# Attention, a token-mixing perceptron and a gated output in float32: three blocks of engine programs joined into one, with the last steps of the attention reordered around the first mixing

## The chip, the cores and the metric

The kernel runs on one core of a Trainium2 chip. The metric is the time of one execution on the device in microseconds (us); lower is better. The engines are named as in the profile: PE (matmuls and transposes), DVE, ACT and POOL for the elementwise work, SP as issuer of most DMAs.

## What is computed

The reference, cut to what matters. Shapes: q, k, v (4, 8, 576, 64), x (4, 576, 512), U (576, 32), V (32, 576), w_ch1 (512, 2048), w_ch2 (2048, 512), w_val and w_out (512, 512), conv_w (5, 512).

```python
scores = q @ k.T / sqrt(64)
scores = where(scores >= max(scores) - tau, scores, -1e9)
attn = exp(scores - max(scores)); attn = attn / (sum(attn) + 1e-9)
x = (attn @ v)                                   # back to (4, 576, 512)

u = x + (x.T @ U @ V).T                          # mixing of the tokens
x = u + maximum(u @ w_ch1, 0) @ w_ch2            # perceptron

gate = sigmoid(sum(conv_w[j] * xp[:, j:j + 576] for j in range(5)))
out = (gate * (x @ w_val)) @ w_out
```

## The kernel before

Everything is float32. A product is made of three matmuls of parts: an operand is split into a high part (rounded to the matmul's format) and a low part (the rest), and high x high, high x low and low x high are added in PSUM. The high parts are casts on ACT, the low parts subtractions on DVE or POOL. The tokens stay transposed on the chip in `x_t`, 128 channels on the partitions in four column blocks d for each of 4 batches. Each batch has two halves of 288 tokens (`CHUNK`).

The kernel is three functions, each with one block of five engine programs. A block ends for all engines together. Every engine runs its own instructions in the order written; between engines there are semaphores (`until` and `wait_ge` wait, `then_inc` counts).

`attention` goes through 80 steps m (`STEPS`: 16 pairs of heads, 5 blocks of query rows: 128, 128, 128, 96, 96) and 160 scores n = 2m, 2m + 1. For a step PE makes the scores (`score_rows`), transposes the weights (`transpose_main(m, a)`, `transpose_tails(m)`) and multiplies them with v (`weigh_values(m)`, L291); ACT makes exponentials (L369) and evacuates the transposes (`evac_main`, L396, `evac_tails`, L402); DVE makes the maximum (L494), the thresholded weights (`weights`, L503) and `normalise(m)` into `x_t` (L516). POOL splits q and k and, one chunk for each pair, makes the low part of w1 (`w1_low`, L227). PSUM has eight banks: scores take banks 0 to 5 in turn, the transposes bank 6, the output of `weigh_values` bank 7.

Behind the last scores comes the drain, L343 to L360 on PE, where the first mixing (batch 0, first half) is woven in: `transpose_tokens(k)` (L304) brings five blocks of tokens of batch 0 into banks 2 to 5 as scores leave them, ACT and DVE split them (`token_high` L412, `token_low` L522), `mix_down(k)` multiplies them with U (`u4_sb`, L315 and L316) into bank 0, `g_high` (L459) and `g_low` (L541) split the result g, `mix_up(d)` (L326) multiplies it with V, `mix_sum(d)` (L548) adds it to x. `u_high` is L463, the low parts of u are made by POOL (L237, d = 0, 1) and DVE (L580, d = 2, 3). `u4_sb` and V (`v4_sb`) are split in the drain too.

`mixing_and_perceptron` has 32 units u for each of the 4 batches, 16 for each half. A unit on PE is `hidden(b, u)` (L721 to L723, 12 matmuls with w1) and `output(b, u - 1)` (L736 to L738, 12 matmuls with w2, `h_used` counts them); `hidden_high` on ACT (L787) and `hidden_low` on DVE (L862) stand between them. Row blocks 0 to 8 of w2 are in `w2a_hi` and `w2a_lo`, the other seven in `w2b_hi` and `w2b_lo`; they are loaded and split one by one in the first 16 units (`w2_high` L799, `w2_low` L875). In the last batch w_val and w_out are split into freed places, and `x_high` (L808) and `x_low` (L888) make the parts of the first two chunks of x. POOL makes the convolution of each chunk (18 steps, L932 and L936) and SP stores it to DRAM (`conv_dram`).

`gated_output` has eight chunks c of 288 tokens. PE runs `value(c)` (48 matmuls, L1005 to L1007) into banks 0 to 3 and then two or three `project(s)` (12 matmuls of 512 columns, L1020 to L1022). SP loads `gates`, ACT makes `sigmoid(c)` (L1055), DVE `multiply(c)` (L1083, four), ACT `gated_high(c)` (L1043), DVE `gated_low(c)` (L1088). `x_high(c + 2)` (L1037) and `x_low(c + 2)` (L1076) prepare the chunk after the next. POOL makes the convolution of the last chunk beside this. On DVE the order of a chunk is:

```python
            for c in range(CHUNKS):
                multiply(c)
                if c + 2 < CHUNKS:
                    x_low(c + 2)
                gated_low(c)
```

## Time and profile before

| | |
|---|---|
| runs shown (3) | 835.25, 836.61, 836.88 us; median 836.61 |
| profiled execution | 835.42 us; span of its instructions 833.6 us |
| granted PE clock, mean over the span | 0.998 |
| busy, share of the span | PE 98%, DVE 53%, ACT 48%, POOL 48% |
| HBM | 38.81 MB read, 8.85 MB written, 57 GB/s over the span |

The span goes from the first to the last instruction of the profiled execution; the execution's own time is 1.8 us longer. The attention takes the first 36% of the span, the perceptron goes to 87%. The page says who is busy, the waits say who waited for whom, the timelines show each instruction with the idle time before it, and the windows show busy time and clock of a stretch. A matmul's recorded duration (0.29 us for 288 columns) is longer than its distance to the next (0.133 us), since matmuls overlap; costs on PE are counted from start to start. "PEq" is PE's sequencer, which is what the waits name where a block begins.

### The profile page before, as it was taken

What the parts mean: (1) busy time and instruction counts of PE and PEld (TensorE: products, weight loads), DVE (VectorE), ACT (ScalarE), POOL (GpSimd) and SP (SyncE); (2) the same over time, 40 slices, a digit from 0 to 9 for tenths busy, and PEclk for the clock granted to TensorE, in tenths of its full rate; (3) what the DMA queues carried; (4) which work ended last, traced back from release to release, by engine and by line L of the source; (5) the groups of instructions that cost most, each with busy time, mean ns of one, the idle gap of its engine ahead of it and who ended that gap; (6) DMA issues with size and microseconds to landing.
All of it is one profiled execution on the core that took longest, in us unless ns stands there. A gap on an engine that the chain in (4) does not pass through costs nothing. (4 is left out here: it accounts for less than half of the span.)

```text
span 833.6 us, 17430 instructions
## 1 busy us (share of the span) xinstructions
PE 812.9 (98%) x6864; PEld 770.5 (92%) x6864; DVE 443.4 (53%) x996; ACT 397.4 (48%) x1019; POOL 396.6 (48%) x290
## 2 busy tenths in 40 slices
PE   4999999999999989999999999999999999999998
PEld 4889888899889879999999999999999999988986
DVE  6999999999999854332231322313223123384231
ACT  5999999999999933222121221212212112244231
POOL 4999887788860000082280731905509147191000
PEclk9999999999999999999999999999999999999999
DMA  7444334333422022100000000000000102122221
GB/s 180 115 128 115 85 110 125 104 85 93 125 64 69 2 64 89 39 1 29 1 29 2 1 29 1 2 29 1 29 2 1 54 25 82 37 104 94 80 79 63
DMA packets 27759, 49.36 MB, mean 59 GB/s; under 512 B 5344, under 2 KB 14112, under 8 KB 27680
## 3 DMA queue, kind: packets, MB, share of 16 engines
q1 hardware_dynamic: 24944, 43.54, 18.5%
q10 hardware_dynamic: 2736, 4.72, 1.5%
q8 instruction: 55, 0.90, 0.4%
q14 instruction: 24, 0.20, 0.1%
HBM read 38.81 MB, written 8.85 MB: 57 GB/s over the span
## 5 line engine op out<-in xcount | busy, mean ns | idle before, releaser
L862 DVE SCALAR_TENSOR_TENSOR h_lo<-psum,h_hi 128x288 fp32r<-128x288 f32 x128 | 58.6, 458 | 244.7 <-ACT h_hi L787 244.7
L787 ACT ACTIVATE h_hi<-psum 128x288 fp32r<-128x288 f32 x128 | 52.7, 412 | 256.0 <-PE psum L723 256.0
L721 PE MATMUL psum<-u_split,w_hi 128*128 128x288 f32 x512 | 152.0, 297 | 3.1 <-PEq L135 3.1
L723 PE MATMUL psum<-u_split,w_lo 128*128 128x288 f32 x512 | 152.3, 297 | 0.0
L722 PE MATMUL psum<-u_split,w_hi 128*128 128x288 f32 x512 | 151.8, 297 | 0.0
L494 DVE TENSOR_REDUCE neg_max<-psum 128x1 f32<-128x576 f32 (+1 forms) x160 | 119.2, 745 | 20.4 <-PE psum L254 20.1
L503 DVE SCALAR_TENSOR_TENSOR probs<-psum,thresh,exp_scores 128x576 f32<-128x576 f32 (+1 forms) x160 | 129.3, 808 | 0.8 <-ACT exp_scores L369 0.8
L932 POOL TENSOR_TENSOR conv<-x_t,cw 128x576 f32<-128x576 f32 x14 | 16.1, 1153 | 232.5 <-DVE x_t L870 231.9
L369 ACT ACTIVATE exp_scores<-psum,neg_max 128x576 f32<-128x576 f32 (+1 forms) x160 | 118.1, 738 | 0.0
L253 PE MATMUL psum<-qk_split 128*128 128x288 f32 (+1 forms) x320 | 105.8, 345 | 10.5 <-DVE qk_split L482 9.6
L721 PEld LDWEIGHTS psum<-u_split,w_hi 128*128 128x128 f32 x512 | 97.1, 190 | 3.9 <-issue 3.3
L722 PEld LDWEIGHTS psum<-u_split,w_hi 128*128 128x128 f32 x512 | 96.9, 189 | 0.7
L723 PEld LDWEIGHTS psum<-u_split,w_lo 128*128 128x128 f32 x512 | 96.9, 189 | 0.0
L254 PE MATMUL psum<-k_lo,qk_split 128*128 128x288 f32 (+1 forms) x320 | 91.5, 300 | 0.0
L396 ACT COPY probs_t<-psum 128x384 f32<-128x384 f32 (+2 forms) x160 | 79.5, 497 | 13.9 <-PE psum L264 12.3
L737 PE MATMUL psum<-h_lo,w2a_hi 128*128 128x288 f32 x288 | 85.1, 296 | 0.0
L736 PE MATMUL psum<-h_hi,w2a_hi 128*128 128x288 f32 x288 | 85.1, 295 | 0.0
L738 PE MATMUL psum<-h_hi,w2a_lo 128*128 128x288 f32 x288 | 85.0, 295 | 0.0
L264 PE MATMUL psum<-ident,probs 128*128 128x128 f32 (+1 forms) x560 | 82.6, 264 | 0.8 <-ACT probs_t L396 0.8
L936 POOL TENSOR_TENSOR conv<-conv,term 128x576 f32<-128x576 f32 x56 | 81.0, 1447 | 4.4
L291 PE MATMUL psum<-probs_t,v_main 128*64 128x128 f32 (+1 forms) x1280 | 80.7, 268 | 0.0
L253 PEld LDWEIGHTS psum<-qk_split 128*128 128x128 f32 (+1 forms) x320 | 58.3, 182 | 23.1 <-issue 16.5
(127 smaller groups left out, 1900.4 us busy)
## 6 DMA issues: line engine op xcount, KB each, us to landing
qk_raw<-in_qk SPq DMA_DIRECT2D x60, 288.0 KB, 4.3
out<-o_sb ACTq DMA_DIRECT2D x18, 256.0 KB, 2.0
w_stage<-in_w SPq DMA_DIRECT2D x16, 256.0 KB, 3.1
v_main<-in_v SPq DMA_DIRECT2D x16, 256.0 KB, 2.6
conv<-in_w SPq DMA_DIRECT2D x16, 256.0 KB, 2.6
conv_dram<-conv SPq DMA_DIRECT2D x7, 576.0 KB, 2.9
gates<-conv_dram SPq DMA_DIRECT2D x7, 576.0 KB, 3.7
probs<-in_qk SPq DMA_DIRECT2D x4, 288.0 KB, 5.0
```

The lines of the kernel that those rows point to most:

```text
L253: nc.tensor.matmul(out, split[:, hd, 0, rows], split[:, hd, 1, cols], start=True, stop=False)
L254: mm = nc.tensor.matmul(out, split[:, hd, 0, rows], k_lo[:, hd, cols], start=False, stop=True)
L264: mm = nc.tensor.transpose(psum[:, T_BANK, kb * P:kb * P + rows], probs[0:rows, m % 3, at:at + P], ident[0:rows, 0:rows])
L369: nc.scalar.activation(halves(e_sb[0:rows, n % 2]), scores(n, rows), ACT.Exp, bias=neg_max[0:rows, n % 5:n % 5 + 1]).then_inc(exp_done, 1)
L494: nc.vector.tensor_reduce(neg_max[0:rows, n % 5:n % 5 + 1], scores(n, rows), AX.XY, ALU.max, negate=True).then_inc(max_done, 1)
L503: nc.vector.scalar_tensor_tensor(out=halves(probs[0:rows, m % 3, n % 2 * S:(n % 2 + 1) * S]), in0=scores(n, rows), scalar=thresh[0:rows, n ...
L721: nc.tensor.matmul(out, w1_hi[:, cols], u_hi[:, half, d], start=(d == 0), stop=False)
L722: nc.tensor.matmul(out, w1_hi[:, cols], u_lo[:, half, d], start=False, stop=False)
L723: mm = nc.tensor.matmul(out, w1_lo[:, cols], u_hi[:, half, d], start=False, stop=(d == DB - 1))
L736: nc.tensor.matmul(out, hi[:, cols], h_hi[:, u % 2], start=(f == 0), stop=False)
L737: nc.tensor.matmul(out, hi[:, cols], h_lo[:, u % 2], start=False, stop=False)
L738: mm = nc.tensor.matmul(out, lo[:, cols], h_hi[:, u % 2], start=False, stop=(f == FB - 1))
```

## The change

- The three functions return their engine programs, and one block runs them one behind the other, so each engine goes on to the next function when it is itself done. Waits that the blocks' ends gave are written out as semaphores.
- In the drain, the token transposes stand ahead of the last steps' transposes; the order on PE, ACT and DVE is new. The last two scores' work on ACT is taken out of the loop. `mix_down` runs in two column halves of 256 into banks 0 and 1, `g_high` and `g_low` likewise, and `mix_up(0)` waits for the first half alone. `hidden(0)` waits for each column block of the low part of u. All low parts of u are made on DVE. `weigh_values(78)` comes behind `mix_up`; `transpose_tails(79)`, `weigh_values(79)`, `evac_tails(79)` and `normalise(79)` go into the first two units of the perceptron.
- U and V are split on POOL, ahead of its last `w1_low`, with products by one in place of ACT's casts. `g4_sb` and `tok_lo` swap their places, the ring of `probs` is shifted by one. The loads of w2 wait for the split of V.
- `gates` lies in the place of the first rows of `w2b_hi`; its first two loads wait until these rows have been used for the last time (`h_used`) and run within the perceptron.
- `value(0)` writes banks 4 to 7, `value(1)` waits for `x2_done`. `gated_high(c)` stands ahead of `x_high(c + 2)` and `gated_low(c)` ahead of `x_low(c + 2)`. POOL's last convolution waits for `x_low(2)`.

The diff, cut to its core; the shift of the bodies' indentation is left out.

```diff
+Programs = namedtuple("Programs", "sync gpsimd tensor scalar vector")
+LastStep = namedtuple("LastStep", "transpose_tails weigh_values evac_tails normalise")
...
     tok_hi, tok_lo = parts[0:5], parts[5:10]
-    X_BANKS, G_BANK = [2, 3, 4, 5, 2], 0
+    X_BANKS, G_BANKS, G_COLS = [2, 3, 4, 5, 2], [0, 1], [slice(0, DM // 2), slice(DM // 2, DM)]
+    U_BANKS = [0, 2, 3, 1]
...
             work(p)
-        for c in (PAIRS - 2, PAIRS - 1):
-            pool.wait_ge(w1_lo_done, c)
-            w1_low(c)
-        for d in (0, 1):
-            pool.wait_ge(u_hi_done, d + 1)
-            nc.gpsimd.tensor_tensor(*low_part_of_u(d), ALU.subtract)
+        pool.wait_ge(w1_lo_done, PAIRS - 2)
+        w1_low(PAIRS - 2)
...
+        pool.wait_ge(mix_in, 16 * 5)
+        pool.wait_ge(w1_lo_done, PAIRS - 1)
+        u_rank, v_rows = slice(0, 3 * RANK), slice(RANK, 2 * RANK)
+        nc.gpsimd.tensor_tensor(u4_sb[:, :, u_rank], u4_raw[:, :, u_rank],
+                                one[:].unsqueeze(2).broadcast_to([P, 5, 3 * RANK]), ALU.mult).then_inc(u4_hi_done, 1)
+        pool.wait_ge(u4_hi_done, 1)
+        nc.gpsimd.tensor_tensor(u4_sb[:, :, 3 * RANK:P], u4_raw[:, :, 3 * RANK:P], u4_sb[:, :, 0:RANK].bitcast(F32),
+                                ALU.subtract).then_inc(u4_ready, 1)
+        pool.wait_ge(u4_ready, 1)
+        nc.gpsimd.tensor_tensor(v4_sb[:], v_stage, one[:].broadcast_to([P, S]), ALU.mult).then_inc(v_hi_done, 1)
+        pool.wait_ge(v_hi_done, 1)
+        nc.gpsimd.tensor_tensor(v4_sb[v_rows], v_stage[v_rows], v4_sb[v_rows].bitcast(F32), ALU.subtract
+                                ).then_inc(v_split, 1)
+        pool.wait_ge(v_split, 1)
+        w1_low(PAIRS - 1)
...
             pe.wait_ge(tok_evac, k + 1)
-            nc.tensor.matmul(psum[:, G_BANK, :], u4_sb[0:rows, k], tok_hi[k][0:rows], start=(k == 0), stop=False)
-            mm = nc.tensor.matmul(psum[:, G_BANK, :], u4_sb[0:rows, k], tok_lo[k][0:rows], start=False,
-                                  stop=(k == 4))
-            if k == 4:
-                mm.then_inc(g_sum, 1)
+            for bank, cols in zip(G_BANKS, G_COLS):
+                out = psum[:, bank, 0:DM // 2]
+                nc.tensor.matmul(out, u4_sb[0:rows, k], tok_hi[k][0:rows, cols], start=(k == 0), stop=False)
+                mm = nc.tensor.matmul(out, u4_sb[0:rows, k], tok_lo[k][0:rows, cols], start=False, stop=(k == 4))
+                if k == 4:
+                    mm.then_inc(g_sum, 1)
...
             if d == 0:
-                pe.wait_ge(g_ready, 1)
                 pe.wait_ge(v_split, 1)
-            nc.tensor.matmul(psum[:, 2 + d, 0:CHUNK], g4_sb[:, d * P:(d + 1) * P], v4_sb[:, 0:CHUNK],
+            pe.wait_ge(g_ready, d // 2 + 1)
+            nc.tensor.matmul(psum[:, U_BANKS[d], 0:CHUNK], g4_sb[:, d * P:(d + 1) * P], v4_sb[:, 0:CHUNK],
                              start=True, stop=True).then_inc(mix_ready, 1)
...
             score_rows(2 * i + 1)
+            if i == STEPS - 1:
+                transpose_tokens(0)
+                transpose_tokens(1)
             if i > 1:
                 transpose_main(i - 2, 1)
-                transpose_tails(i - 2)
+                transpose_tails(pe, i - 2)
             if i + 1 < STEPS:
                 score_rows(2 * i + 2)
+            else:
+                transpose_tokens(2)
+                transpose_tokens(3)
             if i > 0:
...
             if i > 1:
-                weigh_values(i - 2)
+                weigh_values(pe, i - 2)
-        transpose_tokens(0)
-        transpose_tokens(1)
-        transpose_main(STEPS - 2, 1)
-        transpose_tails(STEPS - 2)
-        transpose_tokens(2)
-        transpose_main(STEPS - 1, 0)
-        weigh_values(STEPS - 2)
-        transpose_tokens(3)
-        mix_down(0)
         transpose_tokens(4)
-        mix_down(1)
-        transpose_main(STEPS - 1, 1)
-        transpose_tails(STEPS - 1)
-        for k in (2, 3, 4):
+        mix_down(0)
+        transpose_main(STEPS - 2, 1)
+        transpose_tails(pe, STEPS - 2)
+        for k in range(1, 5):
             mix_down(k)
-        weigh_values(STEPS - 1)
+        transpose_main(STEPS - 1, 0)
         for d in range(DB):
             mix_up(d)
+        weigh_values(pe, STEPS - 2)
+        transpose_main(STEPS - 1, 1)
...
-        for i in range(STEPS):
+        def g_high(c):
+            act.wait_ge(g_sum, c + 1)
+            nc.scalar.copy(g4_sb[:, G_COLS[c]], psum[:, G_BANKS[c], 0:DM // 2]).then_inc(g_hi_done, 1)
+        def u_high(d):
+            act.wait_ge(u_sum, d + 1)
+            nc.scalar.copy(high_part_of_u(d), u_cols(d)).then_inc(u_hi_done, 1)
+        for i in range(STEPS - 1):
...
-        spread_inverse(STEPS - 2)
-        act.wait_ge(mix_in, 16 * 5)
-        nc.scalar.copy(u4_sb[:, :, 0:3 * RANK], u4_raw[:, :, 0:3 * RANK]).then_inc(u4_hi_done, 1)
+        spread_inverse(STEPS - 3)
+        threshold(2 * STEPS - 2)
+        exponent(2 * STEPS - 2)
+        guard_sums(STEPS - 2)
+        w1_high(PAIRS - 1)
         token_high(0)
+        threshold(2 * STEPS - 1)
+        exponent(2 * STEPS - 1)
         token_high(1)
-        evac_main(STEPS - 2, 1)
-        evac_tails(STEPS - 2)
+        evac_main(STEPS - 3, 1)
+        evac_tails(act, STEPS - 3)
         guard_sums(STEPS - 1)
         token_high(2)
-        evac_main(STEPS - 1, 0)
-        spread_inverse(STEPS - 1)
+        evac_main(STEPS - 2, 0)
+        spread_inverse(STEPS - 2)
         token_high(3)
         token_high(4)
-        nc.scalar.copy(v4_sb[:], v_stage).then_inc(v_hi_done, 1)
-        evac_main(STEPS - 1, 1)
-        evac_tails(STEPS - 1)
-        act.wait_ge(g_sum, 1)
-        nc.scalar.copy(g4_sb[:], psum[:, G_BANK]).then_inc(g_hi_done, 1)
+        evac_main(STEPS - 2, 1)
+        evac_tails(act, STEPS - 2)
+        spread_inverse(STEPS - 1)
+        evac_main(STEPS - 1, 0)
+        act.wait_ge(w1_lo_done, PAIRS)
+        g_high(0)
+        g_high(1)
         for d in range(DB):
+            u_high(d)
+        evac_main(STEPS - 1, 1)
...
+        def u_low(d):
+            dve.wait_ge(u_hi_done, d + 1)
+            nc.vector.tensor_tensor(u_split[:, 0, 1, d], u_cols(d), high_part_of_u(d).bitcast(F32),
+                                    ALU.subtract).then_inc(u_low_done, 1)
...
-        weights(2 * STEPS - 1)
-        normalise(STEPS - 3)
-        u4_low()
         token_low(0)
+        weights(2 * STEPS - 1)
         token_low(1)
...
         token_low(2)
-        normalise(STEPS - 2)
+        normalise(dve, STEPS - 3)
         token_low(3)
         token_low(4)
-        v_low()
-        g_low()
-        normalise(STEPS - 1)
-        for d in range(DB):
-            mix_sum(d)
-        for d in (2, 3):
-            dve.wait_ge(u_hi_done, d + 1)
-            nc.vector.tensor_tensor(*low_part_of_u(d), ALU.subtract)
+        g_low(0)
+        g_low(1)
+        mix_sum(0)
+        mix_sum(1)
+        u_low(0)
+        mix_sum(2)
+        u_low(1)
+        mix_sum(3)
+        normalise(dve, STEPS - 2)
+        u_low(2)
+        u_low(3)
...
+    (gates,), (w2b_hi,) = overlay(nc, ctx, [("gates", [P, 2, DB, CHUNK], F32)], [("w2b_hi", [P, FB - FA, DM], F32R)])
...
+    def sync(sp):
+        sp.wait_ge(v_split, 1)
         for f in range(1, FB):
...
                 until(pe, g_ready, b)
+            if b == 0 and d == 0:
+                pe.wait_ge(o_evac, STEPS)
...
             until(pe, h_done, n - 1)
+            if b == 0 and half == 0 and f % DB == 0:
+                pe.wait_ge(w1_lo_done, PAIRS - DB + f // DB + 1)
             out = psum[:, 4 + u % 2, 0:CHUNK]
             for d in range(DB):
+                if n == 0:
+                    pe.wait_ge(u_low_done, d + 1)
...
                 hidden(b, u)
+                if first and u == 0:
+                    last_step.transpose_tails(pe, STEPS - 1)
+                if first and u == 1:
+                    last_step.weigh_values(pe, STEPS - 1)
...
             until(act, w2_in[f % 2], 16 * ((f + 1) // 2))
+            if f == FA:
+                act.wait_ge(o_evac, STEPS)
             nc.scalar.copy(w2_rows(w2a_hi, w2b_hi, f), w2_stage[f % 2]).then_inc(w2_hi_done, 1)
...
                 hidden_high(b, u)
+                if first and u == 0:
+                    last_step.evac_tails(act, STEPS - 1)
...
+        act.wait_ge(mix_in, 16 * 5)
         w2_high(0)
...
                 hidden_low(b, u)
+                if first and u == 1:
+                    last_step.normalise(dve, STEPS - 1)
...
     BLOCKS = B * S // P
+    x2_done, h_used, conv_out, first_x_ready = perceptron_sems
+    VALUE_BANK = [4] + [0] * (CHUNKS - 1)
...
+    def sync(sp):
         for c in range(CHUNKS):
...
             until(sp, gv_part, DB * (c - 1))
+            if c < 2:
+                last_row = ((c + 1) * DB * CHUNK - 1) // DM + FA
+                sp.wait_ge(h_used, (CHUNKS - 1) * (FB - 1) + last_row + 1)
             if c == CHUNKS - 1:
...
             else:
+                sp.wait_ge(conv_out, 16 * (c + 1))
                 sp.dma_start(gates[:, c % 2], conv_dram[c]).then_inc(gate_in[c % 2], 16)
...
+    def gpsimd(pool):
+        pool.wait_ge(x_ready, DB)
+        pool.wait_ge(x2_done, CHUNKS * DB)
         convolution(nc, pool, B - 1, 1, 0, x_t, last_conv, term, cw, conv_step)
...
             for d, k in itertools.product(range(DB), repeat=2):
-                until(pe, x_ready, (c - 2) * DB + k + 1)
-                if k == 0:
-                    until(pe, gv_part, (c - 1) * DB + d + 1)
-                out_ps, cols = psum[:, d, 0:CHUNK], slice(k * DM + d * P, k * DM + d * P + P)
+                if c > 1:
+                    pe.wait_ge(x_ready, (c - 2) * DB + k + 1)
+                else:
+                    pe.wait_ge(first_x_ready, 2 * k + c + 1)
+                if k == 0 and c > 1:
+                    pe.wait_ge(gv_part, (c - 1) * DB + d + 1)
+                if k == 0 and c == 1:
+                    pe.wait_ge(x2_done, (CHUNKS - 1) * DB + d + 1)
+                out_ps, cols = psum[:, VALUE_BANK[c] + d, 0:CHUNK], slice(k * DM + d * P, k * DM + d * P + P)
...
         for c in range(CHUNKS):
+            gated_high(c)
             if c + 2 < CHUNKS:
                 x_high(c + 2)
-            gated_high(c)
...
             multiply(c)
+            gated_low(c)
             if c + 2 < CHUNKS:
                 x_low(c + 2)
-            gated_low(c)
...
+            gated = gated_output(nc, stage, w_val_hi, w_val_lo, (w2a_hi, w2a_lo), cw, conv_dram, out, psum, x_t, gates,
+                                 perceptron_sems)
+            with nc.Block() as block:
+                @block.sync
+                def _(sp):
+                    scores_and_values.sync(sp)
+                    perceptron.sync(sp)
+                    gated.sync(sp)
```

## Rows read from the trace of the kernel before

**Rows 1.** Page, part 1: busy us (share of the span) xinstructions of each engine.

```profile
PE 812.9 (98%) x6864; PEld 770.5 (92%) x6864; DVE 443.4 (53%) x996; ACT 397.4 (48%) x1019; POOL 396.6 (48%) x290
```

**Rows 2.** Waits of PE: line waited for, us in total, times, longest us.

```profile
PE psum L253 <- DVE qk_split L482: 9.6, 2, 8.4
PE psum L721 <- PEq L135: 3.1, 1, 3.1
PE psum L1020 <- DVE gv_lo L1088: 2.0, 1, 2.0
```

**Rows 3.** Timeline, PE, 725 to 742: start us, us, instruction, [idle before <-releaser].

```profile
725.14 0.29 PE L738 MATMUL psum<-h_hi,w2b_lo 128*128 128x288 f32 x1
726.25 0.37 PE L1005 MATMUL psum<-w2a_hi,w_val_hi 128*128 128x288 f32 x1 [0.82 <-PEq L640]
...
738.98 0.29 PE L1007 MATMUL psum<-w2a_hi,w_val_lo 128*128 128x288 f32 x1
741.24 0.50 PE L1020 MATMUL psum<-w2a_hi,gv_hi 128*128 128x512 f32 x1 [1.97 <-DVE gv_lo L1088]
```

**Rows 4.** Timeline, PE, 282 to 304, the drain and the first unit.

```profile
282.62 0.49 PE L264 MATMUL psum<-ident,probs 128*128 128x128 f32 x3
...
289.62 0.48 PE L315 MATMUL psum<-qk_split,u_sb 128*128 128x512 f32 x1
...
290.17 0.60 PE L304 MATMUL psum<-ident,x_t 128*64 128x128 f32 x4
...
293.28 0.88 PE L291 MATMUL psum<-probs_t,v_main 128*64 128x96 f32 x16
...
294.75 0.80 PE L326 MATMUL psum<-v_sb,g_sb 128*128 128x288 f32 x4 [0.42 <-DVE g_sb L541]
298.60 0.37 PE L721 MATMUL psum<-u_split,w_hi 128*128 128x288 f32 x1 [3.06 <-PEq L135]
...
303.39 0.29 PE L736 MATMUL psum<-h_hi,w2a_hi 128*128 128x288 f32 x1
```

**Rows 5.** Windows: us, busy us (x) of PE, PEld, DVE, ACT, POOL, clock, DMA, GB/s.

```profile
284.00:286.00 2.00, 2.00 (x28) 1.71 (x28) 1.35 (x6) 2.00 (x7) 0.77 (x1) 1.00 0.00 0
300.00:301.00 1.00, 1.00 (x6) 1.00 (x5) 0.00 (x0) 0.00 (x0) 0.00 (x0) 0.50 0.82 207
330.00:400.00 70.00, 70.00 (x526) 69.55 (x525) 22.66 (x45) 16.42 (x36) 22.91 (x18) 1.00 0.08 25
```

**Rows 6.** Timeline, DVE, 294 to 298.

```profile
294.00 0.69 DVE L541 TENSOR_TENSOR g_sb<-psum,g_sb 32x512 fp32r<-32x512 f32 x1 [1.12 <-ACT g_sb L459]
...
296.87 1.42 DVE L580 TENSOR_TENSOR u_split<-x_t,u_split 128x288 fp32r<-128x288 f32 x2
```

**Rows 7.** Timeline, POOL, 283 to 298.

```profile
283.49 1.28 POOL L227 TENSOR_TENSOR w_lo<-w_stage,w_hi 128x512 fp32r<-128x512 f32 x1 [15.80 <-ACT w_hi L407]
296.19 1.79 POOL L237 TENSOR_TENSOR u_split<-x_t,u_split 128x288 fp32r<-128x288 f32 x2 [11.42 <-ACT u_split L463]
```

**Rows 8.** Timeline, DVE, 733 to 757.

```profile
733.38 5.59 DVE L1076 TENSOR_TENSOR w2a_lo<-x_t,w2a_hi 128x288 fp32r<-128x288 f32 x4
738.89 2.30 DVE L1088 TENSOR_TENSOR gv_lo<-gv,gv_hi 128x1152 fp32r<-128x1152 f32 x1
...
754.02 1.56 DVE L1076 TENSOR_TENSOR w2a_lo<-x_t,w2a_hi 128x288 fp32r<-128x288 f32 x4
756.08 1.36 DVE L1088 TENSOR_TENSOR gv_lo<-gv,gv_hi 128x1152 fp32r<-128x1152 f32 x1 [0.50 <-ACT gv_hi L1043]
```

**Rows 9.** Timeline, ACT, 293 to 298.

```profile
293.38 0.59 ACT L459 CAST g_sb<-psum 128x512 fp32r<-128x512 f32 x1 [0.84 <-PE psum L316]
295.68 1.52 ACT L463 CAST u_split<-x_t 128x288 fp32r<-128x288 f32 x4 [1.71 <-DVE x_t L548]
```

**Rows 10.** Timeline, ACT, 726 to 731.

```profile
726.50 1.28 ACT L1055 ACT_TABLE_LOAD   x1 [3.14 <-PEq L640]
730.16 1.17 ACT L1055 ACTIVATE gates<-gates 128x1152 f32<-128x1152 f32 x1 [2.38 <-DMA gates<-conv_dram]
```

More of the change, by code:

```diff
@@ new lines, in gpsimd, with convolve, batch @@
+    def gpsimd(pool):
+        def convolve(b, half):
+            c = b * 2 + half
+            if isinstance(b, int) and c == 0:
+                pool.wait_ge(w2_ready, FB)
+            pool.wait_ge(x2_done, c * DB + DB)
+            until(pool, conv_out, c * 16)
+            convolution(nc, pool, b, half, c * CONV_STEPS, x_t, conv, term, cw, conv_step)
+        def batch(b, first, last):
+            if not first:
+                convolve(b - 1, 1)
+                pool.wait_ge(conv_step, b * (2 * CONV_STEPS))
+            convolve(b, 0)
+        batch_loop(batch)
```

1307 lines of the change are left out of this document (643 added, 664 removed).

## The prediction

> **What bounds the kernel now.** I read the page first. PE is busy for 812.9 us of a span of 833.6 [rows 1], so only its idle time and its slow stretches can be won; DVE, ACT and POOL are busy for about half. The waits of PE name the idle time: 3.1 us before the first matmul of the perceptron (L721), 2.0 before the first output projection (L1020) [rows 2], 0.82 before the first value matmul (L1005) [rows 3], 0.42 before the first `mix_up` (L326) [rows 4]. Most of the rest of the span's 20.7 us without PE is the start (8.4 us until the first scores [rows 2]) and the last store, both left alone by the change. The windows show one thing more: just behind the 3.1 us gap the granted clock is 0.50 (1.2 of 2.4 GHz), while it is 1.00 before and later [rows 5]. Then I took the timelines around the two places where one block ends and the next begins, near 295 us and near 725 us; everything the change can move lies there. In between, one unit of the perceptron is 24 matmuls at 0.133 us from start to start (526 in 70 us of an always busy PE [rows 5]), and the change adds nothing to it.
>
> **First place: attention to perceptron.** `output(0)`, the first matmul of w2, starts at 303.39 [rows 4]. I compute when it starts after the change.
>
> Old order. `score_rows(159)` is the last instruction on PE that both orders share; what follows it starts at 282.62 [rows 4]. From there to `mix_up(0)` at 294.75 PE has 12.1 us, of which I add up 10.6 us of work (start to start: 0.33 to 0.46 for a group of transposes, 1.25 or 0.98 for `weigh_values` with 128 or 96 rows, 0.55 for one `mix_down`, 289.62 to 290.17 in [rows 4]) and 1.5 of waits. From `mix_up(0)` to the first matmul of `hidden(0)` are 3.85 us (294.75 to 298.60): DVE and ACT have to make u, its high and its low part for four column blocks, POOL makes two of the low parts while DVE makes the others, and both are slow at it (1.42 us for two on DVE, 1.79 on POOL [rows 6, 7]), where DVE takes 1.56 for four of this shape when POOL rests [rows 8]; then the blocks' barrier, 0.3 us, since DVE ends at 298.29. From 298.60 to `output(0)` are 4.79 us for 24 matmuls. At 0.133 they would take 3.2, or 3.3 with a slow first one; the other 1.5 us are what the low clock costs.
>
> New order. Before `mix_up(0)` PE no longer has `weigh_values(78)` (0.98), `transpose_main(79,1)` (0.25), `transpose_tails(79)` (0.25) and `weigh_values(79)` (0.98): 10.6 - 2.5 = 8.1 us. The ten matmuls of `mix_down` with 512 columns become twenty with 256. Bounds: 0.11 us each (a transpose of 128 columns) to 0.24 (one of 512 columns); I take 0.14, near the 0.133 of 288 columns plus what a change of weights adds in `mix_down` now, so 2.8 us as before (2.2 to 4.7). Waits in the new order: `transpose_tokens(2)` for the weights of score 158 (0.3), `transpose_main(78,0)` for ACT, which now has two `token_high` and one exponential ahead of its evacuation (0.3), a slow first matmul behind each wait (0.3 in all), and the chain ahead of `mix_up(0)`: `evac_main(79,0)` stands in front of `g_high(0)` on ACT (0.37 us from start to start), then the halves of `g_high` and `g_low`. These took 0.59 and 0.69 with 512 columns [rows 6, 9], four casts of 288 took 1.52, so about 0.43 for one; I take 0.43 for each half (0.3 to 0.69), with hops 1.6 us. So `mix_up(0)` starts at 282.6 + 8.1 + 0.9 + 1.6 = 293.2.
>
> From there DVE has the chain: `mix_sum(0)` starts 0.45 later, and eight instructions of 0.37 us from start to start, `normalise(78)` of 0.26 in their midst and a wait of 0.2 for `u_high(0)` end with `u_low(3)` at 297.1; POOL is idle, so none is slowed. PE takes `weigh_values(78)` and `transpose_main(79,1)` (1.2 us) meanwhile and runs the first three quarters of `hidden(0)` as the low parts come, since its waits are now one for each column block. The last three matmuls start at 297.1 and leave PE free at 297.5. `transpose_tails(79)`, `hidden(1)` and `weigh_values(79)` follow (0.25 + 1.6 + 0.98 = 2.8), so `output(0)` starts at 300.3: 3.1 us earlier than 303.39. This counts the clock as kept: no single wait in this stretch is longer than 1.6 us, and the old kernel has one of 1.97 us at 739 with full-speed matmuls behind it [rows 3], while its fall came behind one of 3.06.
>
> Edits at no cost, and their cover. The splits of u4 and v4 leave ACT and DVE for POOL. POOL is idle for 15.80 us ahead of its last `w1_low` [rows 7], and four instructions of 0.5 to 1.4 us each, some 4 us, fit in there; their five loads stand in SP's queue as before, ahead of the last load of w1, and POOL waits for them with nothing but the last `w1_low` queued behind. The last `w1_low` must now be done before ACT's `g_high`: it ends near 285. SP's loads of w2 wait for the split of v4 and so start well before the perceptron. `normalise(79)` stands behind `hidden_low(1)` on DVE and holds back `w2_low(2)` by under 1 us; `output(2)` needs that more than 5 us later. The shifted ring of `probs` moves no instruction.
>
> **Second place: perceptron to gated output.** The last matmul of the perceptron starts at 725.14, the first of `value(0)` at 726.25: 1.11 us, where 0.13 is the pitch. The last of `value(1)` starts at 738.98, `project(0)` at 741.24: 2.26 us, where 0.13 is the pitch [rows 3]. With 0.1 for each slow first matmul, both gaps are 3.2 us. What ends the second is DVE: `x_low(2)` stands ahead of `gated_low(0)`, and POOL's last convolution runs beside them; four `x_low` take 5.59 us and `gated_low` 2.30, where later chunks show 1.56 for the four and 1.36 for `gated_low` [rows 8]. New: `value(0)` writes banks 4 to 7, free once `hidden_low(31)` has read, which the last `output` waits for anyway, so it follows at 725.3 and `value(1)` ends at 738.1. The gates load while PE is in units 12 to 14 (from about 713, some 4 us each), so ACT takes its table (1.28 us) and the first sigmoid (1.17) right behind its last `x_high`; ACT has been idle for 3.14 us at 726.50, so that is from 723.4, and both are done near 726, ahead of the first value block at 727. Now the sigmoid starts at 730.16 [rows 10]. `multiply(0)` ends at 732.3, `gated_high(0)` at 733.5 and, with POOL still waiting for `x_ready`, `gated_low(0)` at 734.9. `project(0)` wants it at 738.1: cover of 3.2 us, both gaps go, 3.2 us.
>
> What comes due later. POOL's 18 steps start near 737 instead of 726 and end near 765, so the slow DVE instructions move into chunks 1 and 2. For a chunk these are 2.6 + 5.7 + 4 x 0.46 = 10.1 us of DVE in 12.0 us of PE; `x_low(3)` ends near 748 and `value(3)` wants it at 756, `x_low(4)` at 760 for 768. Covered by some 8 us; `last_conv` is read only by the last chunk.
>
> **Sum.** 3.1 + 3.2 = 6.3 us. The profiled execution took 835.42 (span 833.6); less 6.3 that is 829.1. The median of the runs is 836.61, 1.2 above the profiled one; by it the time is 830.3. I take 829.8.
>
> **Rivals.**
> - *The clock falls in the drain all the same.* For it: the new order puts six groups of transposes together from 282.6 to 286, and PE then idles in five pieces until 297. Against: the whole attention stage with its transposes is at 1.00, and so is the old drain up to the 3.06 us gap. Price: as now 1.5 us, 831.3. The Trainium skill, "TensorE: Matmul & The Clock Gate", Part 4, says that transposes don't count as busy work for the clock gate as matmuls do; by it this rival would be the forecast and the drain would be slow at that place. Of the trace of before a mixed window bears on it, against the rule: 284 to 286, with value matmuls and token transposes, is at 1.00 [rows 5]; a pure run of transposes of 3 us it does not have. Chance 0.12.
> - *The chain on ACT and DVE eats the gain of the drain.* A half of g or an evacuation costs more than I took, or PE's extra matmuls cost 0.24 each (+1.9 us), and `output(0)` starts only 1 us or less earlier. Only the second place pays: 832. Chance 0.12.
> - *The second place keeps its gap*, because the gates or the semaphores of the last w2 rows come late, or DVE waits for PE at `x2_done`: 2 us back, 831.8. The first sigmoid has 2 to 6 us of cover. Chance 0.06.
> - *Slower.* POOL's later convolution meets DVE where DVE is on PE's path. DVE has 10.1 us of work in 12.0; if each slowed instruction takes twice the 1.4 and 2.6 us, DVE falls 6 to 8 us behind in each of two chunks, its 8 us of cover are gone in the second, and PE loses more than the 6.3 gained: about 838. It decides from some 16 us of DVE a chunk. The price of the slowed instructions is measured beside the same POOL instructions, so it is unlikely. Chance 0.03.
>
> **Chances and range.** The forecast holds 0.67. About 0.2% is what a measurement of this kernel can tell from no change: 1.7 us, and every case but the last is well below 835: faster 0.93, same 0.04 (the first two rivals together with the third), slower 0.03. Low end: the profiled time less both gains, with 1.3 us more from cheaper halves and an earlier u, 827.8. High end: the first and second rivals and some scatter of the runs, 832.6.
>
> **What would show it.** In the profile after: no `PEq` wait before the first w1 matmul; clock 1.00 in each window from 282 to 305; the first `mix_down` halves at 0.14 us; about 1.5 us of PE's wait before the first `mix_up`; `output(0)` near 300.3; no wait of PE between 720 and 745 beyond 0.2 us; the four `x_low` of chunk 2 at 1.6 us and those of chunk 3 at 5.7, with PE unbroken. A slow stretch of matmuls between 286 and 300, or an idle PE at `value(3)`, would make the prediction wrong.

## The result, and the profile after

The changed kernel takes 829.37 us (median of 4 runs, 829.22 to 830.13) against 836.75 us for the kernel before, a ratio of 0.9921 (95% interval 0.9909 to 0.9933). Five more runs on another occasion gave 829.30 (829.24 to 829.33) and a ratio of 0.9924 [0.9911, 0.9936]. The forecast was 829.8, its range 827.8 to 832.6. The span of the profiled execution fell from 833.6 to 827.3, so by 6.3 us, where 6.3 was predicted; 0.2 us of that were there when the scores ended, as shown below.

The page's span and busy line, and then the waits of PE (engine, tensor, line waited at, what ended it, us in total, times, longest), of the changed kernel:

```profile
span 827.3 us, 17448 instructions
...
PE 811.4 (98%) x6874; PEld 769.3 (93%) x6874; DVE 440.8 (53%) x997; ACT 396.1 (48%) x1018; POOL 398.9 (48%) x292
...
engine line waited for: us in total, times, longest us
PE psum L309 <- DVE qk_split L515: 9.6, 2, 8.4
PE psum L355 <- DVE g_sb L556: 1.4, 1, 1.4
PE psum L309 <- DVE probs L536: 0.9, 1, 0.9
PE psum L320 <- DVE probs L536: 0.3, 1, 0.3
PE psum L320 <- ACT probs_t L423: 0.2, 1, 0.2
PE psum L749 <- DVE u_split L561: 0.2, 1, 0.2
```

PE is busy 1.5 us less although it has ten matmuls more, which fits the 1.5 us that the low clock cost before. The waits of 3.1 and 2.0 us [rows 2] are gone; of waits over 1 us only one is left behind the start, 1.4 us ahead of the first `mix_up` (L355).

The first place, PE's timeline from the end of the scores to `output(0)` (start, us, engine, line, operation, tensors, shapes, count, the idle time before and what ended it):

```profile
282.27 0.30 PE L310 MATMUL psum<-k_lo,qk_split 128*96 128x288 f32 x1
282.40 1.04 PE L332 MATMUL psum<-ident,x_t 128*128 128x128 f32 x8
...
287.81 0.28 PE L346 MATMUL psum<-qk_split,u_sb 128*128 128x256 f32 x1
287.92 0.28 PE L345 MATMUL psum<-qk_split,u_sb 128*128 128x256 f32 x1
...
290.87 0.55 PE L320 MATMUL psum<-ident,probs 96*128 96x96 f32 x4
292.81 0.78 PE L355 MATMUL psum<-v_sb,g_sb 128*128 128x288 f32 x4 [1.39 <-DVE g_sb L556]
293.52 0.88 PE L166 MATMUL psum<-probs_t,v_main 128*64 128x96 f32 x16
...
294.78 0.37 PE L749 MATMUL psum<-u_split,w_hi 128*128 128x288 f32 x1
...
296.31 0.41 PE L749 MATMUL psum<-u_split,w_hi 128*128 128x288 f32 x1 [0.23 <-DVE u_split L561]
```

`output(0)` starts at 300.19 (row below), where it was at 303.39 [rows 4]: 3.2 us earlier. The scores ended 0.22 us earlier already (282.40 against 282.62), which is scatter: in the profiles of the two kernels and their variants they end between 282.24 and 282.99. Counted from there, `output(0)` comes after 17.79 us in place of 20.77, so the drain itself gives 2.98. The halves of `mix_down` follow each other at 0.11 to 0.13 us, and at 0.20 behind a change of weights. `hidden(0)` now begins at 294.78, 3.8 us before its old 298.60, and takes its column blocks one by one as `u_low` delivers them.

```profile
300.19 0.40 PE L764 MATMUL psum<-h_hi,w2a_hi 128*128 128x288 f32 x1
```

The windows of that stretch (window, length, busy us and count of PE, PEld, DVE, ACT and POOL, the granted clock, DMA share, GB/s), to be read beside [rows 5], where 300 to 301 stood at 0.50:

```profile
282.00:284.00 2.00, 2.00 (x18) 1.85 (x17) 1.61 (x3) 2.00 (x7) 0.63 (x1) 1.00 0.00 0
284.00:286.00 2.00, 1.65 (x15) 1.24 (x14) 2.00 (x7) 2.00 (x6) 0.65 (x1) 1.00 0.00 0
...
292.00:294.00 2.00, 1.19 (x16) 1.05 (x18) 1.54 (x4) 0.78 (x3) 0.00 (x0) 1.00 0.00 0
294.00:296.00 2.00, 1.99 (x23) 1.49 (x19) 1.87 (x7) 1.17 (x4) 0.00 (x0) 1.00 0.00 0
296.00:298.00 2.00, 1.77 (x14) 1.69 (x14) 1.49 (x4) 1.57 (x5) 0.00 (x0) 1.00 0.00 0
```

The second place: the last matmul of the perceptron (L766), the first of `value(0)` (L1052) and, after the last of `value(1)` (L1054), the first of `project(0)` (L1067). Below them are DVE's `gated_low(0)` (L1133), the `x_low` of chunks 2 and 3 (L1121) and POOL's first step of the last convolution.

```profile
722.05 0.29 PE L766 MATMUL psum<-h_hi,w2b_lo 128*128 128x288 f32 x1
722.19 0.30 PE L1052 MATMUL psum<-w2a_hi,w_val_hi 128*128 128x288 f32 x1
...
734.84 0.29 PE L1054 MATMUL psum<-w2a_hi,w_val_lo 128*128 128x288 f32 x1
734.97 0.40 PE L1067 MATMUL psum<-w2a_hi,gv_hi 128*128 128x512 f32 x1
...
730.45 1.36 DVE L1133 TENSOR_TENSOR gv_lo<-gv,gv_hi 128x1152 fp32r<-128x1152 f32 x1 [1.22 <-ACT gv_hi L1089]
731.72 1.56 DVE L1121 TENSOR_TENSOR w2a_lo<-x_t,w2a_hi 128x288 fp32r<-128x288 f32 x4
...
736.85 1.62 DVE L1133 TENSOR_TENSOR gv_lo<-gv,gv_hi 128x1152 fp32r<-128x1152 f32 x1 [1.23 <-ACT gv_hi L1089]
738.40 5.94 DVE L1121 TENSOR_TENSOR w2a_lo<-x_t,w2a_hi 128x288 fp32r<-128x288 f32 x4
```

Both gaps [rows 3] are at the pitch of the matmuls, 0.13 to 0.14 us. `project(0)` starts 6.27 us earlier than its old 741.24; of that 3.20 were there at `output(0)` (2.98 and the 0.22 from ahead of the drain), and 3.07 come after it.

### The profile page after: what moved, and what is told of

It is laid out like the page before. It is cut to its first block, busy times and chain, and to the rows that moved or that the text cites. A ratio compares the mean times of both kernels' runs of the same rounds, so it can differ in the third digit from the quotient of the medians.

```text
span 827.3 us, 17448 instructions
## 1 busy us (share of the span) xinstructions
PE 811.4 (98%) x6874; PEld 769.3 (93%) x6874; DVE 440.8 (53%) x997; ACT 396.1 (48%) x1018; POOL 398.9 (48%) x292
## 4 chain that ended last, share of the span: by engine, by line
PE 93%; POOL 3%; DMA 1%; DVE 1%; SPq 1%; ACT 0%; issue 0%; POOLq 0%
PE psum L166 10%; PE psum L765 8%; PE psum L764 8%; PE psum L749 8%; PE psum L766 8%; PE psum L751 8%; PE psum L750 8%; PE psum L320 6%; PE psum L309 6%; PE psum L310 4%; PE psum L1052 2%; PE psum L1054 2%; PE psum L1068 2%; PE psum L1053 2%; PE psum L1067 2%; PE psum L1069 2%
## 5 line engine op out<-in xcount | busy, mean ns | idle before, releaser
L971 POOL TENSOR_TENSOR conv<-x_t,cw 128x576 f32<-128x576 f32 x14 | 16.1, 1152 | 242.7 <-DVE x_t L905 242.2
L766 PE MATMUL psum<-h_hi,w2a_lo 128*128 128x288 f32 x288 | 85.0, 295 | 0.0
```

What stands on the lines that cost most here:

```text
L766: mm = nc.tensor.matmul(out, lo[:, cols], h_hi[:, u % 2], start=False, stop=(f == FB - 1))
```

## The experiments

All times are medians; the kernel before, run beside them, had medians of 835.49 to 836.38. A run's list holds the mean granted clock of each execution. It turned out to matter: every one of the 39 executions of the kernel before that ran beside the experiments is below 1.000.

**The order without the join.** The changed programs, run as three blocks instead of one:

```diff
-            with nc.Block() as block:
-                @block.sync
-                def _(sp):
-                    scores_and_values.sync(sp)
-                    perceptron.sync(sp)
-                    gated.sync(sp)
...
+            def run(part):
+                with nc.Block() as block:
+                    @block.sync
+                    def _(sp):
+                        part.sync(sp)
...
+            run(scores_and_values)
+            run(perceptron)
+            run(gated)
```

> The changed kernel with its three programs in three blocks again, every instruction and its order on each engine kept. My reasoning says that joining is worth what PE waits at the two ends. At the first, PE is done with transpose_main(79,1) at 294.8 and could start hidden(0) only when DVE's u_low(3) is done (296.7) plus 0.3 for the barrier, so the 12 matmuls of hidden(0) all come behind 297.0 and output(0) starts some 1.4 us later than 300.2. At the second, PE waits for the last residual and the barrier, 0.8 to 1.0 us. project(0) should wait for nothing. Sum: 2.2 to 2.4 us, span 829.6, time 831.7. The clock should stay at 1.00, since the wait of PE is near 2.2 us. Rival 1: the order is worth nothing without the join, and the time is back at 835. Rival 2: a wait of 2.2 us is enough for the clock to fall, 1.5 us more, 833.2.

Measured: 832.17 us (831.95 to 833.5, 6 runs), ratio 0.9958 [0.9946, 0.9971]. Its waits of PE, and the first `hidden` and `output` matmul:

```profile
PE psum L749 <- PEq L1195: 2.2, 1, 2.2
PE psum L355 <- DVE g_sb L556: 1.4, 1, 1.4
...
PE psum L1052 <- PEq L1195: 0.8, 1, 0.8
```
```profile
297.35 0.37 PE L749 MATMUL psum<-u_split,w_hi 128*128 128x288 f32 x1 [2.21 <-PEq L1195]
...
301.97 0.40 PE L764 MATMUL psum<-h_hi,w2a_hi 128*128 128x288 f32 x1
```

At clock 1.000 (three executions, 831.95 to 832.01) it is 2.7 us behind the changed kernel, 0.3 more than expected. The join pays that: 0.8 us is the wait ahead of `value(0)`, and 1.6 lie between `mix_up(0)` and `output(0)` (8.98 us against 7.38), where one barrier takes the place of four waits; of the remaining 0.3, 0.2 were there when the scores ended. The clock did not stay as expected: three of the six executions are below 1.000, two of them 1.5 us later, which is the second rival in a part of the executions.

**The second place, both edits undone.** `x_high` and `x_low` ahead of `gated_high` and `gated_low` again, and POOL's last convolution not waiting:

```diff
-        pool.wait_ge(x_ready, DB)
...
-            gated_high(c)
             if c + 2 < CHUNKS:
                 x_high(c + 2)
+            gated_high(c)
...
-            gated_low(c)
             if c + 2 < CHUNKS:
                 x_low(c + 2)
+            gated_low(c)
```

> The changed kernel with two edits of the gated output undone: x_high and x_low of the chunk after the next stand ahead of gated_high and gated_low again, and POOL starts its last convolution without waiting for x_low(2). If the wait before project(0) in the kernel before came from these two together, it comes back: multiply(0) ends at 729.2, four x_low take 5.6 us beside POOL and gated_low 2.3, so gated_low(0) ends near 737.1, where PE is free at 735.0: a wait of 2.1 us, span 829.4, time 831.5. Rival: the wait came from the blocks or from the late gates, and with the join and the early gates it does not come back: span 827.3, time 829.4.

Measured: 831.52 us (831.13 to 831.97, 4 runs), ratio 0.9948 [0.9933, 0.9963]; 831.13 and 831.19 at clock 1.000, so 1.8 us above the changed kernel. The wait is back, with 1.5 us where 2.1 were expected, since the four `x_low` took 4.89 us and not 5.6:

```profile
PE psum L1066 <- DVE gv_lo L1132: 1.5, 1, 1.5
```
```profile
730.05 4.89 DVE L1120 TENSOR_TENSOR w2a_lo<-x_t,w2a_hi 128x288 fp32r<-128x288 f32 x4
734.86 2.57 DVE L1132 TENSOR_TENSOR gv_lo<-gv,gv_hi 128x1152 fp32r<-128x1152 f32 x1
```

**Each of the two alone.** Only the order undone (the last two hunks of that diff), and only POOL's wait undone (its first line):

> The changed kernel with only the order of the gated output undone (x_high and x_low ahead of gated_high and gated_low), POOL still waiting for x_low(2). Four x_low run alone in 1.6 us, gated_high is done near 731.8, gated_low(0) near 733.2, and PE wants it at 735.0: no wait, span 827.3. Rival: the order is what carries the gain, and a wait of 1 us or more stands before project(0).

> The changed kernel with only POOL's wait for x_low(2) taken out, so its last convolution starts near 722 us. gated_low(0) then runs beside POOL and takes 2.3 us in place of 1.4: it ends near 732.7, before PE wants it at 735.0; x_low(2) takes 5.6 us and ends near 738.5, before value(2) at 740.6: no wait, span 827.3. Rival: POOL's delay is what carries the gain, and a wait of 1 us or more stands before project(0) or value(2).

Measured, one execution each: 829.34 and 830.48 us. Neither has a wait ahead of `project(0)`. With the old order and POOL at rest, the four `x_low` take 1.57 us and `gated_low(0)` is done at 733.4; with the new order and POOL at work, `gated_low(0)` starts at 731.71 and takes 1.53, with 5.94 for the `x_low` behind it. So either edit closes the gap; only without both is it there. The 1.2 us that the second kernel takes more than the changed one lie elsewhere, in code that both share. Its scores end 0.6 us later (282.99 against 282.40), for which the trace shows no cause; the other 0.7 us are in the drain of attention:

```profile
292.00:294.00 2.00, 0.61 (x4) 0.65 (x4) 0.96 (x3) 1.03 (x3) 0.00 (x0) 0.94 0.00 0
294.00:296.00 2.00, 2.00 (x22) 1.61 (x21) 1.87 (x6) 1.19 (x3) 0.00 (x0) 0.50 0.00 0
296.00:298.00 2.00, 2.00 (x16) 1.89 (x13) 1.43 (x5) 1.39 (x4) 0.00 (x0) 0.71 0.00 0
```
```profile
293.39 1.00 PE L355 MATMUL psum<-v_sb,g_sb 128*128 128x288 f32 x4 [1.39 <-DVE g_sb L556]
...
301.46 0.40 PE L764 MATMUL psum<-h_hi,w2a_hi 128*128 128x288 f32 x1
```

The clock fell there to 1.2 GHz behind the same 1.39 us wait that the changed kernel's profile passes at 2.4 GHz. From `mix_up(0)` to `output(0)` are 8.07 us with the fall and 7.38 without it (292.81 to 300.19), so this fall costs 0.7 us, half of what the fall of the kernel before costs. The profiled execution of the kernel with both edits undone has the same fall in the same place, and also 0.7 us more; none of the profiles has a fall behind the wait at `project(0)`.

**The gates loaded late.** `sp.wait_ge(x2_done, CHUNKS * DB)` ahead of the gates' first loads:

> The changed kernel with the first two loads of the gates held back until the last residual is done, some 11 us later than in the changed kernel. They land near 727, the sigmoid is done near 728.3. multiply(0) can then start 4 us later but still ends with the last block of value(0) at 729.2, so no wait of PE: span 827.3, time 829.3 at a mean clock of 1.000. If that holds, laying gates into the place of w2 has no part in the gain. Rival: the early load carries part of the 3.2 us of the second place, and a wait before project(0) or value(1) is seen.

Measured, one execution: 829.19 us, no new wait of PE. The sigmoid moves to 726.35:

```profile
726.35 1.17 ACT L1102 ACTIVATE gates<-gates 128x1152 f32<-128x1152 f32 x1 [4.80 <-DMA gates<-conv_dram]
```

The loads into freed weights carry nothing of the gain: a sigmoid 4.8 us later does no harm.

**The clock in the kernel before.** Twenty matmuls of 288 columns, whose results nothing reads, behind `mix_up` fill the 3.06 us gap:

```diff
+            pe.wait_ge(w1_hi_done, 1)
+            pe.wait_ge(t_evac, 2 * STEPS)
+            for _ in range(20):
+                nc.tensor.matmul(psum[:, T_BANK, 0:CHUNK], w1_hi[:, 0:P], w1_hi[:, 0:CHUNK], start=True, stop=True)
```

> The kernel before with 20 matmuls more, of 288 columns, whose result nobody reads, behind mix_up(3): they fill 2.7 of the 3.06 us in which PE waits for the parts of u and the barrier. Nothing else is changed. If the low clock behind that wait is what costs 1.5 us, the mean clock is 1.000 in every run, the first 24 matmuls of the perceptron are done 1.5 us earlier, span 832.1, time about 834 with little scatter, where the kernel before has 835.3 to 837.5 and a mean clock of 0.995 to 0.998. Rival: the fall comes from something else than the wait (the load of w2 that starts there, the transposes), and clock and time stay.

Measured: 833.9 us (833.66 to 835.82, 11 runs), ratio 0.9984 [0.9975, 0.9993].

```profile
295.14 2.79 PE L364 MATMUL psum<-w_hi 128*128 128x288 f32 x20
298.39 0.37 PE L725 MATMUL psum<-u_split,w_hi 128*128 128x288 f32 x1 [0.45 <-PEq L135]
...
301.65 0.30 PE L740 MATMUL psum<-h_hi,w2a_hi 128*128 128x288 f32 x1
```

The 24 matmuls of `hidden(0)` take 3.26 us, 0.136 each, where they took 4.79, though no useful work was moved: 1.5 us. (`output(0)` starts 1.7 us earlier, but the scores had ended 0.2 us earlier too.) Six executions stayed at 1.000 (833.66 to 833.90), but five were at 0.997 to 0.998 and 835.31 to 835.82. Fourteen more such matmuls ahead of `project(0)` fill the other gap:

> The kernel before with the 20 filler matmuls in the 3 us gap ahead of the perceptron and 14 more in the 2 us gap ahead of project(0), whose results nothing reads. In the kernel with the first filler alone 5 of 11 executions still had a mean clock of 0.997 to 0.998. Theory (the remaining falls came behind the second gap): every execution at 1.000, near 833.8 us, about 2.8 us below the kernel before. Rival (they sit in the drain of attention, ahead of mix_up, where neither filler stands): again about half of the executions at 0.997 to 0.998 and 835.3 us or more.

Measured: 833.87 us (833.67 to 834.25, 11 runs), ratio 0.9977 [0.9969, 0.9986], ten executions at 1.000 and one at 0.999. None of eleven fell with both gaps filled, and five of eleven with the first one filled. That points to the 1.9 us gap at `project(0)` as the place of the falls that were left; no profile caught one there. The kernel before can be read accordingly: of its 39 executions beside these experiments 22 had 0.997 to 0.998 and 835.2 to 835.8 us, as one fall gives, and 17 had 0.995 to 0.996 and 836.3 to 837.5, as two would. That these are two falls is read from the times and clocks, since the profile of before is one of the first kind, and where the second one stands is open: the next two kernels show the same two kinds without any wait at `project(0)`.

**More wait in the changed kernel.** Four extra copies on ACT ahead of `g_high(0)`:

> The changed kernel with four copies more on ACT, one waiting for the other, ahead of g_high(0): about 1.8 us, so that PE's wait before mix_up(0) grows from 1.4 to about 3.2 us. It makes the wait of the kernel before in the drain of the changed one. If the length of one wait decides on the clock, it falls in every run behind it, and the time is 829.3 + 1.8 + 1.5 = 832.6. Rival: the clock follows something else (the mix of transposes and matmuls), falls as rarely as in the changed kernel, and the time is 831.1.

Measured: 832.14 us (831.61 to 832.89, 4 runs), ratio 0.9958 [0.9943, 0.9974], all four below 1.000. Two are at 0.997 to 0.998 (831.61 and 831.71), two at 0.996 (832.58 and 832.89), where 832.6 was expected for one fall. The wait is 3.01 us; behind it the profiled execution, one of the first two, falls once, and has 8.07 us from `mix_up(0)` to `output(0)` again:

```profile
294.00:296.00 2.00, 1.45 (x22) 1.32 (x24) 1.65 (x5) 0.78 (x3) 0.00 (x0) 0.99 0.00 0
296.00:298.00 2.00, 2.00 (x16) 1.78 (x13) 2.00 (x7) 1.17 (x4) 0.00 (x0) 0.50 0.00 0
298.00:300.00 2.00, 2.00 (x13) 2.00 (x13) 1.12 (x2) 0.89 (x3) 0.00 (x0) 0.66 0.00 0
```

**The mixing in one piece.** Ten matmuls of 512 columns for `mix_down`, one `g_high`, one `g_low`:

```diff
-            for bank, cols in zip(G_BANKS, G_COLS):
-                out = psum[:, bank, 0:DM // 2]
-                nc.tensor.matmul(out, u4_sb[0:rows, k], tok_hi[k][0:rows, cols], ...)
-                mm = nc.tensor.matmul(out, u4_sb[0:rows, k], tok_lo[k][0:rows, cols], ...)
+            nc.tensor.matmul(psum[:, 0, :], u4_sb[0:rows, k], tok_hi[k][0:rows], ...)
+            mm = nc.tensor.matmul(psum[:, 0, :], u4_sb[0:rows, k], tok_lo[k][0:rows], ...)
```

> The changed kernel with mix_down in one piece of 512 columns again (ten matmuls instead of twenty, one g_high, one g_low). Theory (the halves only overlap ACT's and DVE's work on g, PE's time for mix_down is the same either way): without them the chain from the last mix_down to mix_up(0) is g_high 0.59 plus g_low 0.69 plus hops, against now half of g_high and half of g_low plus hops, so PE waits about 0.5 us longer (1.9 instead of 1.4 us) and output(0) starts near 300.7 instead of 300.2: 829.8 us where the clock stays, and the clock falls more often than now (831.3 where it does). Rival (halves cost PE more in fixed costs than they save, 0.56 us per block against 0.44 or less): five blocks are shorter together by 0.3 us or more and the time is 829.3 or less.

Measured: 830.63 us (829.77 to 832.13, 5 runs), ratio 0.9943 [0.9928, 0.9957]; 829.77 and 829.79 at clock 1.000, 830.63 at 0.998, 831.90 and 832.13 at 0.995. The wait ahead of `mix_up(0)` is 1.94 us:

```profile
293.49 0.76 PE L353 MATMUL psum<-v_sb,g_sb 128*128 128x288 f32 x4 [1.94 <-DVE g_sb L553]
```

The halves save 0.5 us at an equal clock, all of it in that wait; PE's own time for a block of `mix_down` is the same, 0.55 and 0.56 us from start to start for the first one.

**The same kernel again.** The changed kernel, five executions:

> The changed kernel as it is, run again, for the count of executions in which the granted clock falls. Theory (the fall depends on PE's idle time in the drain and on chance): most executions at 1.000 and 829.2 to 829.5 us, one in four or so at 0.997 to 0.998 and 830 to 831. Rival (the falls in the one-look kernels with the same drain were due to their edits): every execution at 1.000 and within 829.2 to 829.5.

Measured: 829.30 us (829.24 to 829.33), all five at 1.000. With the first four, one execution of nine fell (830.13, at 0.998), 0.8 us above the others.

**A shorter chain.** `g_high` ahead of `evac_main(79, 0)` on ACT, and `normalise(78)` behind `u_low(3)` on DVE:

```diff
-        evac_main(STEPS - 1, 0)
         act.wait_ge(w1_lo_done, PAIRS)
         g_high(0)
         g_high(1)
+        evac_main(STEPS - 1, 0)
...
-        normalise(dve, STEPS - 2)
         u_low(2)
         u_low(3)
+        normalise(dve, STEPS - 2)
```

> The changed kernel with two moves in the drain: g_high(0) and g_high(1) stand ahead of evac_main(79,0) on ACT, and normalise(78) stands behind u_low(3) on DVE. If the chain from g to u_low(3) sets when output(0) starts, the first move brings mix_up(0) 1.1 us forward (ACT takes g_high(0) at 290.75, when the last matmul of the first half is done, in place of 291.83), the second another 0.16: output(0) near 299.0, span 826.1, time 828.1 in executions whose mean clock is 1.000. With less waiting of PE in the drain its clock should also fall more rarely than in the changed kernel (one timed run of four there had a mean clock under 1.000). Rival: PE's own work is the bound of the drain, and nothing moves: 829.4.

Measured: 828.35 us (828.02 to 828.67, 4 runs), ratio 0.991 [0.9896, 0.9923], all four at 1.000: the fastest kernel of the study.

```profile
291.60 0.78 PE L355 MATMUL psum<-v_sb,g_sb 128*128 128x288 f32 x4 [0.35 <-DVE g_sb L556]
...
298.98 0.40 PE L764 MATMUL psum<-h_hi,w2a_hi 128*128 128x288 f32 x1
```

## Why the prediction was right, step by step

**The first place.** `mix_up(0)` was put at 293.2 behind a wait of 1.6 us; it came at 292.81 behind 1.39. Half of that difference lay ahead of the drain already (the scores end at 282.40, not 282.62 [rows 4]); the rest is in that wait, and with it in the halves of g: I took 0.43 us for each on both engines, where ACT's two took 0.65 together (row of ACT, below) and DVE's two 0.76. The halves of `mix_down` were taken at 0.14, inside bounds of 0.11 to 0.24, and came at 0.12 with 0.20 for the first behind a change of weights. `output(0)` was put at 300.3 and came at 300.19. The forecast of 3.1 us less is met by 2.98 counted from the end of the scores; 1.53 of them are the clock and 1.45 moved work. That the total came out at 6.3, as forecast, needed the 0.22 us from ahead of the drain, which is luck. That the chain on ACT and DVE would eat the gain (832) did not happen. ACT's and DVE's rows of g:

```profile
291.83 0.65 ACT L448 CAST g_sb<-psum 128x256 fp32r<-128x256 f32 x2
...
292.24 0.76 DVE L556 TENSOR_TENSOR g_sb<-psum,g_sb 32x256 fp32r<-32x256 f32 x2 [3.06 <-ACT g_sb L448]
```

**The second place.** The prediction worked here with the old times, which the first place shifts by 3.1 us. With that shift it put the end of `gated_low(0)` at 731.8 and `project(0)` at 735.0; they came at 731.81 and 734.97. The sigmoid was put at 722.9, less the same shift, and ended at 722.75. The cover was 3.2 us by the one and by the other. The gain is 3.07 against 3.2; the 0.1 us is lost on the way there: from `output(0)` to `value(0)` are 422.00 us (300.19 to 722.19), and were 421.88 without the gap (303.39 to 726.25, less 1.11 - 0.13). What the prediction did not say is that the two edits which protect `gated_low(0)` are one too many: either alone does it.

**What comes due later.** The four `x_low` of chunk 2 were expected at 1.6 and those of chunk 3 at 5.7; they took 1.56 and 5.94. I counted `gated_low` beside POOL at 2.6, its worst row (2.59 at 748.21; [rows 8] shows only the one of 2.30); in the new order it took 1.62 and 1.65. A chunk's DVE work beside POOL is 9.3 us (1.62 + 5.94 + 0.81 + two of 0.46), not 10.1. PE has no wait from 700 to the end, so the slower case (838) did not come.

**The clock** is where the argument was too simple. The price of 1.5 us was right for the old drain: filling the gap gave 1.53. For the new one, which is what the rival was about, it was twice too high: a fall behind `mix_up(0)` costs 0.69 us in all four profiles that have one (8.07 or 8.08 against 7.38). I read the difference so, though no run separates it: at full clock PE waits for `u_low` in this stretch (matmuls start 0.30 and 0.52 us behind the one before them at 295.42 and 296.31, where the pitch is 0.13), and slow matmuls fill a part of that. The changed kernel's one execution with a fall took 830.13, not the rival's 831.3. And "no single wait in this stretch is longer than 1.6 us" was no reason for safety. Share of executions below 1.000, beside PE's longest waits in the drain:

| kernel | waits of PE in the drain, us | below 1.000 |
|---|---|---|
| before | 0.42, 3.06 | 39 of 39 |
| four copies more | 3.01 | 4 of 4 |
| three blocks | 1.39, 2.21 | 3 of 6 |
| mixing in one piece | 1.94 | 3 of 5 |
| changed kernel | 1.39 | 1 of 9 |
| its drain, only the gated output edited | 1.39 | 3 of 7 |
| shorter chain | 0.35 | 0 of 4 |

Between the ends it differs from execution to execution of the same code, and the 0.12 of that rival was fair by luck. The row next to the last puts together the four kernels with both edits undone (2 of 4; it also has the 1.5 us wait at `project(0)`), POOL early (1 of 1), DVE's old order (0 of 1) and late gates (0 of 1). With the changed kernel these are 4 of 16, and with so few executions neither their 3 of 7 against 1 of 9 nor the 0 of 4 of the shorter chain tells a difference from chance. The other reason against the rival held: sixteen token transposes and ten others between 282.4 and 286 stand in windows at 1.00. The Trainium skill's rule ("TensorE: Matmul & The Clock Gate", Part 4) that transposes don't count as busy for the clock gate the way matmuls do is not borne out by them, but not disproved for a longer run either: the clock was at 1.00 before them, and value matmuls follow at 285.98. The falls that the profiles show all stood behind waits.

**The sum.** The prediction gave 829.1 from the profiled execution and 830.3 from the median, 1.2 us above it, and took 829.8 between them. The profiled execution after took 829.22. The term that was mis-sized is that offset: I treated the 1.2 us as a scatter of which half would stay. It goes with the mean clock instead: the executions of before at 0.995 to 0.996 stand about 1.2 us above those at 0.997 to 0.998, and none of the changed kernel's nine is that low. A second fall, behind the gap at `project(0)`, would do this, and the falls that the second filler took away (5 of 11, then 0 of 11) speak for it. It is not shown: those falls cost 1.5 to 2.0 us and not 1.2, and the kernels with four copies more and with the mixing in one piece have no wait at `project(0)` and yet have executions at 0.995 to 0.996, 0.9 to 1.5 us above their own at 0.997 to 0.998. So the second fall can also be one more in the drain, which the change shortened too. Either way, the 1.97 us wait with full-speed matmuls behind it [rows 3], which was used against the first rival, was one execution and shows only that the clock can pass such a wait. By medians the change gained 7.4 us at first, and 6.2 in the later set, since before's median falls now among the executions of the slower kind (836.75), now among those of the faster (835.49).

**Where the gain comes from,** at clock 1.000 throughout: from 833.8 (both gaps filled) to 829.3 are 4.5 us; undoing the join costs 2.7, undoing the second place's edits 1.8, and 2.7 + 1.8 = 4.5. Nothing is left for the new order of the drain by itself: counted from the end of the scores, `output(0)` comes after 19.38 us in three blocks and 19.25 in the old order with the gap filled. So moving `weigh_values(79)` and the transposes behind `hidden` pays here only together with the join, which brings it to 17.79. What the join would give with the old order was not run, so how the 1.6 us divide between the two stays open. The rest is the clock: some 1.6 us in every execution of before (833.8 to 835.4), and 1.2 more in nearly half of them.

## What to carry to other kernels

- Moving PE's work behind a chain of other engines and removing the barrier behind it are one edit: price them together. Here the first gave nothing alone.
- Where PE bounds a kernel, read the mean granted clock of every execution beside its time. A second cluster of times at a lower clock here meant that a wait was paid twice in part of the executions, once as idle time and once as slow matmuls; one profile shows only one of the cases. What the slow matmuls cost depends on whether PE bounds the stretch: 1.5 us in the old drain, 0.7 in the new one.
- Take an offset between the profiled execution and the median as something with a cause before it is carried over to the forecast.

## What the runs showed of the hardware

A wait of PE of 1.4 to 2.2 us can cost the clock or not, for the same code. None of 0.35 us did in four executions; behind those of 3.0 us no execution kept 1.000 (43 of 43, of which two were profiled). The fall comes behind the wait, and not always at once: with the 3.01 us wait, matmuls start at 294.55 and the windows are at 1.00 or nearly until 296, then at 0.50. A fall costs 1.53 us where PE had nothing to wait for in the stretch behind it, and 0.69 where it had.

DVE's subtraction with both inputs in SBUF takes 1.56 us for four of 288 columns while POOL rests and 5.94 beside POOL's convolution, so 1.48 each, which is about one of POOL's instructions (1.25 and 1.52 us at that time). POOL's own grow by about 0.1 us beside them (1.15 to 1.25, 1.43 to 1.52). Beside one long instruction of 1152 columns it is the other way round: DVE pays 0.3 us (1.62 and 1.65 against 1.36), and POOL's instruction at that time takes 1.0 us more (2.15 in place of 1.15, 2.43 in place of 1.43). In another order DVE took 2.57 for it. The Trainium skill, "SBUF — State Buffer", section "Who interferes with whom", describes an exclusive lock on a port pair shared by the two; that one engine stands while an instruction of the other runs agrees with it in both cases.
